# Attention and two mixtures of layers on one core: loads of queries and keys moved ahead of weights, two tiles of each block left in their products' banks, and other orders around the first block

## The reference

```python
attn = softmax(mask(q @ k.T / 8)) @ v     # 2 batches, 8 heads, 576 tokens, head 64
# heads 0-3: a band of 32 tokens; heads 4-7: every 32nd token
x = attn                                   # 1152 tokens x 512
h = np.maximum(x @ w_in, 0.0)              # 512 -> 2048
x = h * h @ w_out                          # 2048 -> 512
p = domain_probs / (domain_probs.sum(-1, keepdims=True) + 1e-09)
for e in range(4):                         # four experts, 512 -> 1024 -> 512
    h = np.maximum(x @ w1[e], 0.0)
    out += p[:, e:e + 1] * (h @ w2[e])
```

## Time and profile before

| | us |
|---|---|
| median of 3 runs | 630.53 |
| fastest and slowest | 630.06, 632.12 |
| the profiled execution | 632.91 |
| its span (first to last instruction) | 631.1 |
| PE busy in it | 617.3 |

### The profile page before, as it was taken

One profiled execution on the slowest core, in us unless ns is written; L12 is line 12 of the kernel. 1 busy time (PEld: TensorE's weight loads), 2 busy tenths in 40 slices (PEclk: granted clock), 3 DMA queues, 4 the chain that ended last, 5 costly groups with the idle time before them and its releaser, 6 DMA issues.

```text
span 631.1 us, 11318 instructions
## 1 busy us (share of the span) xinstructions
PE 617.3 (98%) x4182; PEld 574.4 (91%) x4182; DVE 381.3 (60%) x995; ACT 246.9 (39%) x666; POOL 295.7 (47%) x251
## 2 busy tenths in 40 slices
PE   8889999999999999999999999999999999999998
PEld 7778999999999999989889889889889889989987
DVE  5797559567576597865465465465465456456452
ACT  7797756343353352641331331332232232232210
POOL 4898875453253258595173173173263263260200
PEclk9999999999999999999999999999999999999999
DMA  8550402021021021022012022021021021020012
GB/s 294 178 149 2 134 2 68 1 68 68 1 68 68 1 68 68 2 67 69 1 67 68 1 68 68 1 68 68 1 68 66 1 74 61 1 68 1 0 51 100
DMA packets 16774, 35.87 MB, mean 57 GB/s; under 512 B 2896, under 2 KB 3664, under 8 KB 16720
## 3 DMA queue, kind: packets, MB, share of 16 engines
q1 hardware_dynamic: 16576, 34.96, 16.6%
q10 hardware_dynamic: 144, 0.20, 0.1%
HBM read 32.79 MB, written 2.36 MB: 56 GB/s over the span
## 4 chain that ended last, share of the span: by engine, by line
PE 89%; DVE 4%; ACT 2%; POOL 2%; issue 1%; DMA 1%; SPq 0%; DVEq 0%; ACTq 0%; POOLq 0%
PE ps L1203 29%; PE ps L1205 28%; PE ps L1204 28%; PE ps L1144 2%; DVE prob L780 1%; PE ps L1200 1%; PE ps L1192 1%; POOL xf_lo L506 1%; DVE probT L800 1%; POOL wb_lo L472 1%; DMA k_buf<-in_k 1%; PE ps L1166 1%; DVE ps L934 0%; ACT prob L572 0%; DVE h_lo L947 0%
## 5 line engine op out<-in xcount | busy, mean ns | idle before, releaser
L1203 PE MATMUL ps<-xf_hi,wa_hi 128*128 128x288 f32 x672 | 199.3, 297 | 0.3 <-DVE u L894 0.3
L1204 PE MATMUL ps<-xf_lo,wa_hi 128*128 128x288 f32 x672 | 198.3, 295 | 0.0
L1205 PE MATMUL ps<-xf_hi,wa_lo 128*128 128x288 f32 x672 | 197.6, 294 | 0.0
L472 POOL TENSOR_TENSOR wb_lo<-raw_b,wb_hi 128x512 fp32r<-128x512 f32 x48 | 60.8, 1298 | 175.3 <-ACT wb_hi L601 175.3
L1203 PEld LDWEIGHTS ps<-xf_hi,wa_hi 128*128 128x128 f32 x672 | 126.0, 188 | 1.3 <-ACT wa_hi L592 0.7
L1204 PEld LDWEIGHTS ps<-xf_lo,wa_hi 128*128 128x128 f32 x672 | 126.2, 188 | 0.5
L1205 PEld LDWEIGHTS ps<-xf_hi,wa_lo 128*128 128x128 f32 x672 | 126.5, 188 | 0.0
L1203 PE MATMUL ps<-wb_hi,h_hi 128*128 128x512 f32 (+1 forms) x292 | 112.9, 387 | 0.4 <-POOL wb_lo L472 0.4
L1205 PE MATMUL ps<-wb_hi,h_lo 128*128 128x512 f32 (+1 forms) x292 | 113.0, 387 | 0.0
L1204 PE MATMUL ps<-wb_lo,h_hi 128*128 128x512 f32 (+1 forms) x292 | 113.0, 387 | 0.0
L976 DVE SCALAR_TENSOR_TENSOR y<-ps,p_norm,y 128x512 f32<-128x512 f32 (+1 forms) x64 | 47.5, 743 | 95.7 <-PE ps L1205 95.7
(11 more groups left out here) (85 smaller groups left out, 875.1 us busy)
## 6 DMA issues: line engine op xcount, KB each, us to landing
raw_a<-in_wa SPq DMA_DIRECT2D x48, 256.0 KB, 3.8
raw_b<-in_wb SPq DMA_DIRECT2D x24, 512.0 KB, 4.9
result<-y SPq DMA_DIRECT2D x8, 256.0 KB, 2.0
q_buf<-in_q SPq DMA_DIRECT2D x7, 288.0 KB, 5.2
k_buf<-in_k SPq DMA_DIRECT2D x7, 288.0 KB, 5.5
v_loc<-in_v_near SPq DMA_DIRECT2D x4, 384.0 KB, 4.7
v_str<-in_v_far SPq DMA_DIRECT2D x4, 320.0 KB, 6.3
result<-y SPq DMA_DIRECT2D x2, 128.0 KB, 1.7
```

The source lines that it names most:

```text
L472: nc.gpsimd.tensor_tensor(wb_lo[:, :, cols], raw_b[:, :, cols], wb_hi[:, :, cols].bitcast(F32), ALU.subtract).then_inc(s_wb_lo, 1)
L1203: nc.tensor.matmul(dst, a_hi, b_hi, start=first, stop=False)
L1204: nc.tensor.matmul(dst, a_hi, b_lo, start=False, stop=False)
L1205: return nc.tensor.matmul(dst, a_lo, b_hi, start=False, stop=last)
```

## The change

Seven edits, in the order of time:

1. SP issues the queries and keys of pairs 2 and 3 before the values of pair 0 and before `load_a(0)`, and those of pair 4 before the values of pairs 2 and 3.
2. POOL makes the remainder of weight form 5 after `x_low(0, 4)` and no longer with pair 4.
3. The form T3 of block 0 is made by DVE after T4 with pair 6 and no longer after the last reciprocal of pair 7; in its place DVE makes the remainder `x_low(0, 2)`, which POOL made between the two halves of pair 7. POOL waits for it before `x_low(0, 3)`.
4. Around B0, the 8 copies to `y` move from ACT to DVE; `x_high(1, 0)` goes after the tile C22; DVE makes the sum of C12 before the remainders of C22, and squares C11 before the second half of `second_sum`.
5. In all blocks but 1 and 8, the tiles C22 and C12 stay in the banks of M5 and M3. Their `c_block` no longer waits on a remainder; M1 and M2 of the next block wait on the remainders of C22 and C12 instead of on their sums.
6. `second_sum` of blocks 2 and 9 is done before the remainders of C12 of blocks 1 and 8.
7. The second weights of block 8 are rounded by ACT within A8 and no longer within A9; POOL makes two of their four remainders between those of x and no longer all after them.

```diff
         def hbank(t, q, u):
-            return (BBANK if t in (1, BLOCKS1) and q % 2 else HBANK) + u
+            if t in (1, BLOCKS1):
+                return (BBANK if q % 2 else HBANK) + u
+            return bank(t, M5, u) if q == C22 else bank(t, M3, u) if q == C12 else HBANK + u
...
             load_qk(0)
             load_qk(1)
+            load_qk(2)
+            load_qk(3)
+            load_a(0)
             load_v(0)
-            load_qk(2)
             load_v(1)
-            load_a(0)
-            load_qk(3)
+            load_qk(4)
             load_v(2)
             load_v(3)
-            load_qk(4)
             load_v(4)
...
-            WA_WITH = {2: [0, 1], 3: [2, 3], 4: [4, 5]}
+            WA_WITH = {2: [0, 1], 3: [2, 3], 4: [4]}
...
-                    if n == NP - 1 and h == 0:
-                        x_low(0, 2)
...
-            for k in (3, 4, 5):
+            pool.wait_ge(s_xf_lo, 3)
+            for k in (3, 4):
                 x_low(0, k)
-            wa_low(0, 6)
-            x_low(0, 6)
+            for k in (5, 6):
+                wa_low(0, k)
+                x_low(0, k)
...
-                if kind == "B" and t in (BLOCKS1 - 2, BLOCKS1 - 1):
+                if kind == "B" and t == BLOCKS1 - 2:
                     for k in range(FORMS):
-                        x_low(t - BLOCKS1 + 4, k)
+                        x_low(2, k)
+                if kind == "B" and t == BLOCKS1 - 1:
+                    for k in (0, 1):
+                        x_low(3, k)
+                    for d in (0, 1):
+                        wb_low(MOE1_SUBS, d)
+                    for k in range(2, FORMS):
+                        x_low(3, k)
+                    for d in (2, 3):
+                        wb_low(MOE1_SUBS, d)
...
-            x_high(1, 0)
             rectified(0, C22)
             squared(0, C22)
             h_high(0, C22)
-            y_copy(0)
-            x_high(1, 1)
+            x_high(1, 0)
             rectified(0, C12)
-            y_copy(1)
             squared(0, C12)
             h_high(0, C12)
-            x_high(1, 2)
-            for k in (2, 3, 4, 5):
-                y_copy(k)
-                x_high(1, k + 1)
-            y_copy(6)
-            y_copy(7)
+            for k in range(1, FORMS):
+                x_high(1, k)
...
+            def x_low(i, k):
+                c = i % 2
+                dve.wait_ge(s_xf_hi, FORMS * i + k + 1)
+                dve.wait_ge(s_xf_lo, FORMS * i + k)
+                nc.vector.tensor_tensor(xf_lo[:, c, k, :, :], t_form[:, c, k, :, :], xf_hi[:, c, k, :, :].bitcast(F32),
+                                        ALU.subtract).then_inc(s_xf_lo, 1)
...
-                elif t in (1, BLOCKS1) and q > C21 or t in (2, BLOCKS1 + 1) and q == C11:
+                elif t in (1, BLOCKS1) and q > C21 or q == C11:
                     dve.wait_ge(s_h_lo, tile_count(t, q, u) - 4)
-                else:
+                elif q == C21:
                     dve.wait_ge(s_h_lo, tile_count(t, q, u) - 2)
...
-                    t_forms(0, T4)
-                if n == NP - 1:
-                    t_forms(0, T3)
+                    t_forms(0, T4, T3)
+            x_low(0, 2)
...
-                    if k == M1 and t > 0:
-                        pe.wait_ge(s_u, 6 * t - 2 + u + 1)
-                        pe.wait_ge(s_c, tile_count(t - 1, C22, u))
-                    elif k == M2 and t > 0:
-                        pe.wait_ge(s_c, tile_count(t - 1, C12, u))
+                    if k in (M1, M2) and t > 0:
+                        last = C22 if k == M1 else C12
+                        if t - 1 in (1, BLOCKS1):
+                            pe.wait_ge(s_u, 6 * t - 2 + u + 1)
+                            pe.wait_ge(s_c, tile_count(t - 1, last, u))
+                        else:
+                            pe.wait_ge(s_h_lo, tile_count(t - 1, last, u))
```

More of the change, by code:

```diff
@@ L550, in _ @@
                 if kind == "A" and t % 2 == 1:
-                    if t > 1:
+                    if t not in (1, BLOCKS1 + 1):
                         for d in range(KT):
@@ L615, in x_high @@
                 nc.scalar.activation(xf_hi[:, c, k, :, :], src, ACT.Copy).then_inc(s_xf_hi, 1)
-            def y_copy(i):
-                dt, half = y_place(0, i)
-                act.wait_ge(s_b, i + 1)
-                nc.scalar.activation(y[:, dt, half * HT:(half + 1) * HT], ps[:, BBANK + i % 2, 0:HT], ACT.Copy)\
-                    .then_inc(s_y, 1)
             def first_product(t):
@@ L738, in _ @@
                     h_high(t, C11)
+                    for d in range(KT):
+                        wb_high(s, d)
                     x_high(3, 3)
@@ L746, in _ @@
                     continue
-                if t % 2 == 1:
+                if t % 2 == 1 and t != BLOCKS1 + 1:
                     for d in range(KT):
@@ L1009, in _ @@
                 c_block(0, C11, u)
-            for u in range(2):
-                second_sum(0, u)
+            second_sum(0, 0)
             for u in range(2):
                 square(0, C11, u)
+            second_sum(0, 1)
             for u in range(2):
@@ L1026, in _ @@
             for u in range(2):
+                c_block(0, C12, u)
+            y_tile(0, 0)
+            for u in range(2):
                 h_low(0, C22, u)
-                c_block(0, C12, u)
+            y_tile(0, 1)
             for u in range(2):
                 h_low(0, C12, u)
+            for i in range(2, 2 * KT):
+                y_tile(0, i)
             for at, (kind, t) in enumerate(ORDER[2:], 2):
@@ L1040, in _ @@
                             c_block(t, C11, u)
-                    for u in range(2):
-                        second_sum(t, u)
+                    if t not in (2, BLOCKS1 + 1):
+                        for u in range(2):
+                            second_sum(t, u)
                     if t == BLOCKS1:
@@ L1079, in _ @@
                                 square(t, C12, u)
+                        for u in range(2):
+                            second_sum(t + 1, u)
                         for u in range(2):
```

## The result

| | before | after |
|---|---|---|
| median, us | 630.37 (4 runs) | 623.85 (4 runs) |
| fastest and slowest | 630.06, 632.12 | 623.67, 624.20 |
| the profiled execution | 632.91 | 623.67 |
| its span | 631.1 | 621.9 |

The ratio is 0.9892, with a 95% interval from 0.9873 to 0.9910: the changed kernel is 6.5 to 6.8 us faster, where 5.3 were forecast. In a second comparison it was 0.9879 [0.9858, 0.9899], with medians of 631.91 and 623.90; three of the seven executions of the kernel before had a mean granted clock of 0.997 there, and all of the changed kernel 1.00. The two profiles have spans 9.2 us apart, so 2.4 to 2.7 us of their difference have to be explained by something that is not in the medians of the first comparison.

The account below looks back on a forecast made before the run. PE was taken as the bound, busy without a break in the steady part, so only its waits could be won. Terms 1.8 + 1.4 + 0.6 + 0.6 + 0.4 + 0.5 = 5.3 us gave 625.2 us, range 623.7 to 627.8.

Parts of the forecast that it names:

- the term of edit 5: B2, B4 and B6: PE's wait at tile 4 goes, 3 x 0.2 = 0.6 us, bounds 0 and 0.7.
- Edit 1, 1.8: Scores of pair 3: PE's wait for their keys goes, 1.8 us, bounds 0.8 and 1.85.
- Edits 2 and 3, 1.4: End of attention: PE's wait before the last `outputs` goes, 1.4 us, bounds 0.6 and 1.55.
- Edit 4, 0.6: Around B0: PE's waits behind ACT's copies to `y` shrink, 0.6 us, bounds 0.3 and 0.95.
- Edits 6 and 7, 0.9: M4 of A2, PE's wait for `second_sum`: 0.4 us; start of B8, its wait for POOL's last weight remainder: 0.5 us.
- PE's busy time: Sign over the whole kernel: PE's busy time stays at 617 within 2 us.
- (a): Loads: values or weights land late, attention moves by 0.8 us only, giving 626.2 us; chance 0.12.
- (b): End of attention: DVE and POOL meet at 54.4, POOL first; moving T3 gives 0.6, so 626.0 us; chance 0.14.
- (c): Attention: ACT or POOL bounds it from 20 us on, the load order gives nothing, 627.0 us; chance 0.07 with (e).
- (d): M1 and M2 in 21 blocks: late remainders cost 0.3 us each, giving 631 us or more; chance 0.03.
- (e): Scores of pair 3: PE did not wait for the keys, load order gives 0, 627.0 us; chance 0.07 with (c).
- The clock: Stretch at 1.2 GHz in 30 to 60 us, worth 1.4 us: kept either way in the range, not the sum.

Follow-up runs that it names:

- e_no1: The changed kernel with SP's loads put back in their old order; measured 624.88 us.
- e_keyslate: The changed kernel with pair 3's queries and keys issued after the first weights and the values of pairs 0 to 3; measured 630.63 us.
- e_before: The kernel before, unchanged, run once more for its profile and the granted clock of each execution; measured 630.59 us, ratio 0.9971.
- e_only1: The kernel before with only the new order of SP's loads; measured 629.69 us, ratio 0.9966 to the kernel before.

## Where the prediction failed: the term of edit 5

The step that failed is edit 5's term, "3 x 0.2 = 0.6", with its upper bound of 0.7: the waits put back cost 2.1 us, and edit 5 alone shortened the stretch from A1 to A8 by 1.98. The change was worth 1.2 to 1.5 us more than forecast, and this term is off by 1.5. The mechanisms of the other terms held, with sizes off by 0.1 to 0.8. That the total still came so near is luck: edit 1, 0.8 too large for the medians, made up for half of edit 5.

- **Edit 1, 1.8.** Keys as the cause: right, by e_no1 and e_keyslate. Against the profile of before the changed kernel and edit 1 alone both won 1.89, the medians 1.0 and 1.1. The term held against the profile it was read from, and was 0.7 to 0.8 us too large for the median that it was used for; why is open. The two late loads behaved as bounded: weights at 15.36, within 14.2 to 16, behind cover; the values in good time.
- **Edits 2 and 3, 1.4.** Right in the part that was worked out: remainder 0.73 us, last `outputs` without a wait, POOL as the next limit at M3 with 0.07 against 0.1. Two errors offset each other. What was won at the last `outputs` is 1.84, because the wait for M2 left slack that came back there, and the new wait took 0.60 first. Against e_before, where no stretch at the lower clock lies between, it is 1.96 and 0.50, and with edit 2's 0.22 the three make 1.68: the 1.7 that the median loses when both edits are undone. "Free" was wrong for edit 2, and the new wait was not foreseen: I priced what comes into T3's old place and not T3 in its new one. Rows of before had the price (1.98 us where it meets POOL), and POOL has its multiplication after every reciprocal.
- **Edit 4, 0.6.** Too small. The wait that I expected to stay, the copy of tile 2 ending 0.2 us late, is there (0.21 us from start to start at 68.73), but costs 0.08 us beyond the normal 0.134 and 0.08 on the matmul behind it; I had charged twice that and more. 1.09 from before to after, 0.8 when it is undone, by profile and median.
- **Edit 5, 0.6: the failed step.** "Term: 3 x 0.2 = 0.6" took 0.2 us for each of B2, B4 and B6, and "In the other blocks PE does not wait for DVE there, so they give nothing". It was worth 1.8 to 2.1. In the even blocks the wait costs 0.35 and not 0.2: 0.22 at the wait, 0.08 at the matmul behind it, and 0.06 at a smaller break earlier in the block. In B1, B3 and B5 PE does lose, 0.45, 0.2 and 0.2 us with the waits put back. In B3 and B5 these are breaks of 0.10 us, 0.24 from start to start, which no row of PE itself marks. The waits of PE's weight loads in the trace of before did name them, behind DVE's instructions at the end of B's tiles, in B1 (L961) and in B3 and B5 (L963):

```profile
PEld ps L1203 <- DVE y L963: 0.3, 2, 0.2
PEld ps L1203 <- DVE y L961: 0.3, 2, 0.2
```

I had priced the rows with a break that is large enough to be marked on PE, and looked neither at these nor at distances between starts. The upper bound of 0.7 was built on the same three blocks, so the range did not hold it either. The mechanism, a wait of DVE on itself costing it 0.1 us a time, was right, for a wait on the instruction directly ahead. The rule weighed against it (the Trainium skill, "VectorE: DVE Perf Modes", The DRAIN you can't avoid) would have given 0; 0.49 against 0.36 us and +2.1 us decide against it here.
- **Edits 6 and 7, 0.9.** 1.0 to 1.1: right within 0.2. Edit 6 takes away a loss of 0.44 as forecast, but 0.15 of it came back behind it, and edit 7 was worth 0.7 for 0.5, above its upper bound.
- **PE's busy time** was to stay at 617 within 2 us. It fell to 612.2, as told above: it takes in short waits and slower matmuls, and is no measure of work.
- **Rivals.** (a) Half true by the medians, not by the reason given: in the changed kernel the values were in time and the late weights covered. In e_only1 the weights were too late to be. (b) did not happen at 54.4; the same collision happened at 45.8. (c) is excluded: delays of 2.3 and 5.0 us put into attention stay whole to the end. (d) did not happen: from A1 on the only break of more than 0.21 us at an M1 or M2 is that of block 2 at 88.35, 0.27 us from start to start, and it was as long before. (e) is excluded.
- **The clock.** Kept out of the sum with the words that the change leaves that pause of PE as it is. Nearly so: it is 1.07 us at 45.39 before and 0.88 at 42.96 after. But the same pause, 1.06 us in e_before, brought no stretch at the lower level there: some executions have one and some not. All eight executions of the changed kernel have a clock of 1.00, and those of the kernel before go as low as 0.987. Which of the edits does that is open: with edit 1 alone two of twelve were below 1.00, with edit 1 undone one of six, with edits 2 and 3 undone two of six. It moves the slowest executions and hardly the median of the first comparison, so most of it does not show in the result.

By the profile of before the terms came to 7.2 us instead of 5.3: 1.89 + 1.24 + 1.09 + 1.83 + 0.44 + 0.69. The start of the program, the clock and edit 2 make it 9.2. Against e_before they are 1.75 + 1.68 + 1.09 + 1.81 + 0.44 + 0.77 = 7.5, and 0.2 of start make the 7.7 between the spans. That is 1 us above the 6.5 measured; that most of it is the part of edit 1 which the medians don't show is likely, and not shown. The measured 623.85 lies at the low end of the range, 623.7, and only by the 0.8 us that the range had for the clock and the spread: the terms with their upper bounds ended at 624.5.

## What to carry to other kernels

Where a matrix engine is nearly always busy, sum what is lost from the distances between the starts of its instructions, not from the rows that name a wait: here 33 distances above normal between 60 and 260 us held 4.2 us, and the waits marked on PE's matmuls in that stretch 0.8. Those marked on its weight loads come to 3.2, so read them too. When an instruction is moved, price it in its new place by the row in which it meets the same neighbour, before pricing what takes its old one. And put the small loads that the first phase waits for ahead of the large ones: it wins the wait, and it takes away a pause behind which the clock can fall.

## What the runs showed of the hardware

- A load that is late for PE has a second price: behind a pause of 3.29 us 18 to 22 us ran at 0.5 to 0.6 of full clock in the profile, and all 12 executions showed a clock below 1.00; with the pause filled with matmuls none of 12 did. Shorter pauses bring it in some executions and not in others: behind one of 2.51 us before the scores of pair 3 the clock was 0.66 from 15 to 30 us, behind one of 1.82 it was 1.00; and behind the pause of 1.07 us at the end of attention 46 to 50 us ran at 0.5 to 0.6 in one profile of the kernel before, and at 1.00 in the other.
- A wait of PE costs 0.08 us beyond its length: the matmul behind the one that waited follows after 0.21 us, not 0.134 (128x288).
- An instruction of DVE that waits for the one directly ahead of it in DVE's stream starts 0.11 to 0.13 us later than one that doesn't (0.48 and 0.49 against 0.37 and 0.36 from start to start, 128x288 in PSUM).
- Where a form or remainder of 128x576 on DVE meets a multiplication of 126x504 on POOL, the one that comes second pays: at 50.46 DVE came first and took 0.73, as alone, and POOL's took 1.46 for 1.02; at 45.78 POOL's was under way and DVE's took 1.59. The Trainium skill ("SBUF — State Buffer", the list on how engine and DMA ports can contend) has a lock that the first to start holds for its whole instruction. The trace agrees: POOL's multiplication ended at 46.76, and DVE's form at 47.37, 0.6 us later, where it takes 0.73 alone.
